# Attention stage: the second half of each token group scaled by ScalarE a head at a time, and one row moved by a transfer

## What is computed

```python
kv  = einsum('bhsd,bhse->bhde', k, v)
out = einsum('bhsd,bhde->bhse', q, kv)
rms = sqrt(mean(out * out, axis=-1, keepdims=True) + 1e-06)   # one per token and head
x   = out / rms * g_norm                                      # [8, 576, 512]
X   = fft(fft(x, axis=1), axis=2);  u = x + real(X)           # head of the second stage
# then twice: u + relu(norm(u) @ w1) @ w2, the second time after a rank-32 mix over the tokens
```

## Time and profile before

| | us |
|---|---|
| median of 3 runs (lowest, highest) | 1857.5 (1851.31, 1861.46) |
| the profiled execution, its whole time | 1865.05 |
| its span in the profile | 1862.7 |
| busy in the span: PE, DVE, ACT, POOL | 1752.5, 1387.9, 783.9, 604.2 |

### The profile page before, as it was taken

One profiled execution on the slowest core, in us unless ns is written; L12 is line 12 of the kernel. 1 busy time (PEld: TensorE's weight loads), 2 busy tenths in 40 slices (PEclk: granted clock), 3 DMA queues, 4 the chain that ended last, 5 costly groups with the idle time before them and its releaser, 6 DMA issues.

```text
span 1862.7 us, 25843 instructions
## 1 busy us (share of the span) xinstructions
PE 1752.5 (94%) x9908; PEld 1681.7 (90%) x9908; DVE 1387.9 (75%) x1559; ACT 783.9 (42%) x1126; POOL 604.2 (32%) x428
## 2 busy tenths in 40 slices
PE   5989868979999999999999999799999999999998
PEld 5767758969999999999999999789999999999998
DVE  3899975897797787877866768965956857758667
ACT  1333333634443544544444436334334434443442
POOL 2888862453041231330320213620410402303203
PEclk9999988989999999999999999899999999999999
DMA  7557548898688787787876778786676766766663
GB/s 251 182 196 237 195 155 315 307 336 295 246 299 273 258 298 270 280 290 257 295 257 232 255 244 316 285 299 221 247 241 232 240 234 245 249 226 240 228 247 122
DMA packets 123819, 470.04 MB, mean 252 GB/s; under 512 B 12273, under 2 KB 49649, under 8 KB 84018
## 3 DMA queue, kind: packets, MB, share of 16 engines
q1 hardware_dynamic: 122482, 467.21, 71.1%
q10 hardware_dynamic: 1216, 1.18, 0.2%
HBM read 389.70 MB, written 78.64 MB: 251 GB/s over the span
## 4 chain that ended last, share of the span: by engine, by line
PE 72%; DVE 15%; issue 5%; POOL 3%; DMA 3%; SPq 0%; ACT 0%; ACTq 0%; DVEq 0%; POOLq 0%
PE pair L837 11%; PE pair L839 11%; PE pair L838 11%; PE pair L854 11%; PE pair L856 11%; PE pair L855 10%; DVE t_raw L1366 3%; DVE t_lo L1347 2%; PE tr_ps L721 2%; DMA in_sb<-x_dram 1%; POOL x_sb L1527 1%; DVE eo_sb L1238 1%; DVE ce_sb L1246 1%; PE pair L628 1%; DVE ss_sb L1212 1%
## 5 line engine op out<-in xcount | busy, mean ns | idle before, releaser
L854 PE MATMUL pair<-t_hi,w_sb 128*128 128x384 f32 x1344 | 462.8, 344 | 33.8 <-DVE t_lo L1347 33.7
L837 PE MATMUL pair<-t_hi,w_sb 128*128 128x384 f32 x1344 | 462.4, 344 | 15.6 <-DVE h_sb L1384 8.3
L855 PE MATMUL pair<-t_lo,w_sb 128*128 128x384 f32 x1344 | 458.2, 341 | 0.0
L856 PE MATMUL pair<-t_hi,w_sb 128*128 128x384 f32 x1344 | 458.1, 341 | 0.0
L838 PE MATMUL pair<-t_lo,w_sb 128*128 128x384 f32 x1344 | 457.3, 340 | 0.0
L839 PE MATMUL pair<-t_hi,w_sb 128*128 128x384 f32 x1344 | 457.2, 340 | 0.0
L1347 DVE TENSOR_TENSOR t_lo<-t_raw,t_hi 128x768 fp32r<-128x768 f32 x300 | 346.4, 1162 | 11.0 <-ACT t_hi L1067 7.6
L1572 POOL TENSOR_TENSOR t_raw<-h_sb 128x768 f32<-128x768 f32 x60 | 150.4, 2507 | 573.7 <-PE pair L856 573.7
L1082 ACT ACTIVATE t_hi<-t_raw 128x768 fp32r<-128x768 f32 x240 | 202.1, 846 | 314.9 <-DVE t_raw L1366 236.4
L854 PEld LDWEIGHTS pair<-t_hi,w_sb 128*128 128x128 f32 x1344 | 254.6, 189 | 42.6 <-DVE t_lo L1347 42.3
L837 PEld LDWEIGHTS pair<-t_hi,w_sb 128*128 128x128 f32 x1344 | 254.0, 189 | 23.7 <-issue 14.1
(11 more groups left out here) (149 smaller groups left out, 2115.8 us busy)
## 6 DMA issues: line engine op xcount, KB each, us to landing
w_sb<-wc SPq DMA_DIRECT2D x260, 1024.0 KB, 4.9
wc<-w_sb SPq DMA_DIRECT2D x28, 1024.0 KB, 5.8
w_raw<-wr1a SPq DMA_DIRECT2D x24, 512.0 KB, 4.9
w_raw<-wr1b SPq DMA_DIRECT2D x24, 512.0 KB, 4.2
wc<-pb SPq DMA_DIRECT2D x16, 640.0 KB, 4.8
w_raw<-wr2a SPq DMA_DIRECT2D x10, 1024.0 KB, 7.0
wc<-pb_v SPq DMA_DIRECT2D x16, 640.0 KB, 4.8
w_raw<-wr2b SPq DMA_DIRECT2D x10, 1024.0 KB, 7.2
```

Of the source, the lines that this page charges most:

```text
L837: nc.tensor.matmul(ps, w_hi, hi[:, x, :], start=(fresh and x == 0), stop=False, skip_group_check=True)
L854: nc.tensor.matmul(ps, w_hi, hi[:, f, :], start=(fresh and k == 0 and f == 0), stop=False, skip_group_check=True)
L855: nc.tensor.matmul(ps, w_hi, lo[:, f, :], start=False, stop=False, skip_group_check=True)
L856: last = nc.tensor.matmul(ps, w_lo, hi[:, f, :], start=False, stop=(k == 3 and f == 1), skip_group_check=True)
```

## The change

Of each group's two members DVE scales only the first (m = 0). The second is scaled by ACT with eight instructions, one for each head: 96 partitions by 64 columns from PSUM to SBUF, a copy whose scale is one column of `rinv_sb`, one value for each partition. They stand in ACT's queue as `normalise(b, g)`: for g = 0 between `copy_seq` 0 and 1, for g = 1 behind root 1, for g = 2 behind root 2 and ahead of `copy_kv`. Their first instruction waits for the reciprocal (`inverted`). The semaphore `scaled` becomes two, `scaled_dve` and `scaled_act`, and all who waited for the one wait for both, but for PE's sine slot 1, which waits for DVE's alone.

The copy of the middle row (L1249) leaves DVE. ACT issues a transfer of it from `x_sb` to `mrow_sb` (`save_row`, 2 KB, SBUF to SBUF) behind `copy_g`, once `weigh` of group 0 is done; `fix_row` and the first `add_transform` of that batch wait for its landing. In batch 0, `save_row` stands ahead of `copy_kv(1)`.

```diff
             def attention(...):
                     if g == 0 and not first:
-                        pe.wait_ge(scaled, 6 * b)
+                        pe.wait_ge(scaled_dve, NT * b)
+                        pe.wait_ge(scaled_act, NT * b)
...
                     if g == 2:
-                        pe.wait_ge(scaled, 6 * b + 2)
+                        pe.wait_ge(scaled_dve, NT * b + 1)
+                        pe.wait_ge(scaled_act, NT * b + 1)
...
+            def normalise(b, g):
+
+                act.wait_ge(inverted, NT * b + g + 1)
+                if b >= 3 and g == 0:
+                    act.wait_ge(u_stored[b % 3], 16 * NT * (b // 3))
+                for h in range(H):
+                    cols = slice(HD * h, HD * (h + 1))
+                    last = nc.scalar.activation(x_sb[b % 3][:, 2 * g + 1, cols], att_ps[2 * (g % 2) + 1][0:PT, cols],
+                                                ACT.Copy, scale=rinv_sb[:, g % 2, H + h:H + h + 1])
+                last.then_inc(scaled_act, 1)
+
+            def save_row(b):
+
+                act.wait_ge(x_ready, NT * b + 1)
+                if b >= 2:
+                    act.wait_ge(row_fixed, b - 1)
+                act.dma_start(mrow_sb[:, b % 2, :], x_sb[b % 3][0:1, 1, :]).then_inc(row_saved[b % 2], 16)
...
                 root(b, 0)
-                copy_seq(b - 1, (0, 1))
+                copy_seq(b - 1, (0,))
+                normalise(b, 0)
+                copy_seq(b - 1, (1,))
                 root(b, 1)
+                normalise(b, 1)
                 copy_seq(b - 1, (2, 3))
                 copy_g(b - 1)
+                save_row(b)
                 if not first:
                     split_unit_hi(UNITS[b - 1])
                 square(b, 2, False)
                 if more:
                     root(b, 2)
+                    normalise(b, 2)
                     copy_kv(b + 1)
...
-                for m in range(2):
-                    nc.vector.tensor_tensor(
-                        x_sb[b % 3][:, 2 * g + m, :].rearrange("p (h e) -> p h e", h=H),
-                        att_ps[2 * (g % 2) + m][0:PT, :].rearrange("p (h e) -> p h e", h=H),
-                        rinv_sb[:, g % 2, H * m:H * (m + 1)].unsqueeze(2).to_broadcast([PT, H, HD]),
-                        ALU.mult).then_inc(scaled, 1)
+                nc.vector.tensor_tensor(
+                    x_sb[b % 3][:, 2 * g, :].rearrange("p (h e) -> p h e", h=H),
+                    att_ps[2 * (g % 2)][0:PT, :].rearrange("p (h e) -> p h e", h=H),
+                    rinv_sb[:, g % 2, 0:H].unsqueeze(2).to_broadcast([PT, H, HD]), ALU.mult).then_inc(scaled_dve, 1)
...
                 if g == 0:
-                    nc.vector.tensor_copy(mrow_sb[:, b % 2, :], x_sb[b % 3][0:1, 1, :])
...
             def fix_row(b):
                 dve.wait_ge(u_added, NT * b + 1)
+                dve.wait_ge(row_saved[b % 2], 16 * (b // 2 + 1))
...
             def weigh(b, g):
                 pool.wait_ge(gn_loaded, 16)
-                pool.wait_ge(scaled, 2 * (NT * b + g + 1))
+                pool.wait_ge(scaled_dve, NT * b + g + 1)
+                pool.wait_ge(scaled_act, NT * b + g + 1)
...
             def add_transform(b, t):
                 pool.wait_ge(ds_ready, NT * b + t + 1)
+                if t == 0:
+                    pool.wait_ge(row_saved[b % 2], 16 * (b // 2 + 1))
```

More of the change, by code:

```diff
@@ L306, in build_program @@
         att_done, squared, summed, eps_set = sem("att_done"), sem("squared"), sem("summed"), sem("eps_set")
-        rooted, inverted, scaled, x_ready = sem("rooted"), sem("inverted"), sem("scaled"), sem("x_ready")
+        rooted, inverted, x_ready = sem("rooted"), sem("inverted"), sem("x_ready")
+        scaled_dve, scaled_act, row_saved = sem("scaled_dve"), sem("scaled_act"), [sem(f"row_saved{n}") for n in range(2)]
         eo_ready, folded = sem("eo_ready"), sem("folded")
@@ L694, in feature_transform @@
                     if t == 1:
-                        pe.wait_ge(scaled, 6 * b + 10 if more else 6 * B)
+                        pe.wait_ge(scaled_dve, NT * (b + 1) + 2 if more else NT * B)
                     elif t or not first:
@@ L774, in up_room @@
                         pe.wait_ge(kv_copied, 2 * B)
-                        pe.wait_ge(scaled, 6 * B)
+                        pe.wait_ge(scaled_dve, NT * B)
+                        pe.wait_ge(scaled_act, NT * B)
                     elif k == 1:
@@ L1023, in _ @@
             root(0, 0)
+            normalise(0, 0)
             root(0, 1)
+            normalise(0, 1)
+            save_row(0)
             copy_kv(1)
@@ L1027, in _ @@
             root(0, 2)
+            normalise(0, 2)
             def deviation(n):
```

## The result

The kernel with the change took 1870.38 us (median of 8 runs, 1867.66 to 1875.44), the kernel before, on the same chips, 1857.59 (8 runs, 1851.31 to 1864.27). The ratio is 1.0073, with an interval of 1.0054 to 1.0093: the change makes the kernel slower by 12.8 us, where +5.7 was forecast. The time lies above the 1858 to 1869 that the forecast itself was given, in the range of 1848 to 1877 and on the slower side of the 0.5% that can be told, a side that had 0.34. The profiled execution took 1873.11, against 1865.05 before.

A forecast was written before the change was run, and what follows sets the result against it. DVE was taken as full in the attention part but held twice a step by a chain through ACT and POOL. Terms of 4.65, 0.42 and 0.60 gave +5.7 us, from 1857.5 to 1863.2, range 1848 to 1877.

The forecast's parts named there:

- PE as the bound or more stalls: Slower case: PE's slow clock delays key-value products, 1875, or DVE stalls in three steps more, 1869; chance 0.26.
- the forecast's own: The main case, a time of 1858 to 1869 us around the sum's 1863.2; chance 0.52.
- the middle row: Row copy moved from DVE to an ACT-issued transfer: -0.42 us a step, with ACT's issue of about 0.67 taken as covered.
- The price of ACT's copies: Each 96x64 copy 0.32 us long and 0.21 from start to start; eight end 1.79 after the first starts.
- Group 0: `weigh` 0 starts later behind ACT's eight copies, +0.51 us a step; DVE's saved 1.28 falls into its wait for POOL.
- Group 1: `copy_seq` 1 waits behind the eight copies, PE runs 2.3 us late, and `weigh` 1 is still on time.
- three signs of being wrong: Copies closer than 0.15 us apart, no DVE idle before L1259, or PE, not ACT, releasing the cosine copies at half clock.
- PE becomes the bound: Rival: a 1.2 GHz stretch on the key-value products delays unfold 0 about 3 us; four steps, +12, 1875; chance 0.26 with more stalls.
- Group 2: Eight copies ahead of `copy_kv` and the cosine copies: unfold 0 starts 0.84 us later, and DVE waits 1.48 there.
- The sum: Five usual steps of +0.93, step 2 +0.42, batch 0 +0.60, last step 0.0: +5.7 us, giving 1863.2.
- DVE's time comes free: Faster rival: 18.7 us leave DVE; were all of it on the path, 1838.8; chance 0.14 together with fewer stalls.
- It doesn't do what it says: Rival: the eight ACT copies cost only the lower bound, so the stage keeps its length or gains a little, 1852; chance 0.08.

The follow-up runs named there:

- g2: The changed kernel without the row's transfer, so DVE copies the row again and ACT keeps the eight copies: 1867.85 us, 1.0050 of before.
- f3: The changed kernel with ACT's `copy_seq` of token slots 1 and 2 each one place earlier, slot 1 ahead of group 0's eight copies: 1864.72 us, 1.0031 of before.
- g7: The changed kernel with DVE scaling both members again and ACT making its eight copies beside that on a scratch area, same waits: 1870.67 us, 1.0085 of before.
- g8: The changed kernel with extra PE matmuls of 200 columns ahead of token slots 1 and 2, their results overwritten: 1870.75 us, 1.0073 of before.
- h1: The kernel before with the row's transfer added into a scratch row, with all its waits, DVE's own copy kept and used: 1862.05 us, 1.0031 of before.
- h3: The changed kernel with ACT's copies of token slots 1 and 2 moved earlier and the row copied by DVE, without the transfer: 1867.28 us, 1.0054 of before.
- g0: The kernel before, unchanged, profiled once more for a second trace: 1862.49 us in that execution.
- f1: The kernel before with only the row's transfer, issued by ACT, in place of DVE's copy; scaling stays on DVE: 1862.61 us, 1.0027 of before.
- h2: The kernel before with only the row's transfer in place of DVE's copy, measured a second time: 1860.91 us, 1.0021 of before.

## Why the prediction was right or wrong, point by point

**The time.** The change came out in the range, but 7.1 us over the sum, in the part that was kept for PE as the bound or more stalls (0.26) and not in the forecast's own (0.52). By the timed halves one term of the sum makes up that distance, the middle row: -3.4 forecast, +4 to +5.5 measured. The scaling alone costs what was forecast for it, 9.3 against 9.1. That agreement is partly luck, as the terms in it were not all right: the stalls were as in before in the forecast, and g2's trace has two more of them.

**The price of ACT's copies: right.** 0.32 long and 1.79 for eight were forecast, 0.312 and 1.72 measured. The trace agrees with the forecast's own rows more than with the 0.33 and 0.24 that were estimated from the Trainium skill (ScalarE: Activation LUTs, What ACT_TABLE_LOAD costs): (1.72 - 0.312) / 7 is 0.20 from start to start. The rule of the Trainium skill (ScalarE: Activation LUTs, Rules for kernel authors) to multiply on VectorE bears out here in sign: g2, the move alone, is +0.5%.

**Group 0: right.** `weigh` 0 was forecast 4.4 to 4.5 after the first sums and starts at 4.41; this is POOL's timeline of step 3 of the kernel after.

```profile
117.39 6.40 POOL L1560 TENSOR_TENSOR x_sb<-x_sb,gn_sb 96x256 f32<-96x256 f32 x8 [1.28 <-ACT x_sb L953]
```

DVE's L1268 follows 7.21 after the first sums, before it was 6.75: +0.46, forecast +0.51. The saving of 1.28 is gone, as said: in g7 DVE gets its 15.4 us back, and the medians differ by 0.3, with the interval of 6.5 to each side.

**Group 1: wrong in steps without a stall.** "In a step without DVE's 4 us stall ACT is there 1.93 earlier, at 153.9, and PE isn't: the two come out level." A lateness of 2.3 used up all of PE's room, and nothing was left over for what came with it: PE's new pause ahead of slot 3 is followed in the trace by a stretch at 1.2 GHz (0.50 from 117.57 to 127.00, stage mean 0.88, 0.91 before), and in step 3 the matmuls got some 5 us longer by it (3.25 - 1.73, 2.95 - 1.62, 3.71 - 1.97 and 6.33 - 5.98, the last two by f3's rows). So PE was not level in unstalled steps but late: they take 29.6 to 31.8, forecast 28.7. f3 takes PE's lateness away and gets the forecast step, 28.3 to 28.6. The clock goes with the pauses in these traces, 0.92 in g8 where they are filled and 0.94 in f3 where two copies come earlier, but g8's time stayed, so what the clock alone is worth is open. Of the prediction's three signs of being wrong this is the third, and it came: in step 3 PE, with a stretch at half clock behind it, releases the copies ahead of unfold 0. The rival "PE becomes the bound" named this mechanism and its price; its chance of 0.26 was too low for a case in which the forecast's own working ended with no margin.

**Group 2: right for ACT, short for PE.** Forecast 1.48 of waiting at unfold 0; ACT's own part is 1.81 (f3, g2), the change has 1.8 to 3.6.

**The middle row: the failed term, wrong in sign.** It was set to -0.42 a batch, -3.4 in all, with the issue at nothing. In the traces a step does get 0.27 shorter. In the timed runs three kernels with the transfer cost 4.1, 5.5 and 5.3 us, by h1 because of what was added: 7.5 to 8.9 us beside the forecast, as much as the whole sum missed. Where these us go is open. The traces can't say it: the two of before are of executions 5 and 7.5 us over its median, so nearly every kernel looks as if it lost more in the timed runs than its stage explains. Counted from the span's start to the end of the stage, against the mean of the two traces of before (252.9), ten of the twelve other kernels (all but the change and g7) lose 3 to 7 us more in the timed ratio than in the trace, and g2 and h3, which have no transfer, are among them (4.8 and 5.9).

**The sum.** By batches the change's stage grew +0.6, +2.6, -0.7, +4.1, +1.4, +1.2, +2.0 and -0.8 against the first trace of before, 10.4 in all. The forecast had +0.6, then five of +0.93, +0.42 and nothing for the last. Batch 0 is right from its first sums on, but these come 1.9 us later, which was not forecast. The surplus lies where the step is without a stall: steps 1, 3, 5 and 6 grew by 9.8, against 3.7 forecast (step 6 of before was a stalled one). That is the account of one trace against one, and it doesn't add to that of the timed halves: by the trace the surplus is PE's, by the timed runs it is the row's, and f3's gain speaks for PE. How the two share it is open. The shift was carried on one for one. In the profiled runs the stage ended 12.3 later and the span only 8.6, since the rest of the span varies by some 5 us between traces whatever the kernel (1604.8 to 1610.1 in most, see the table), so single spans could not settle it.

**DVE's time comes free: fell.** It lost 26.7 us of busy time and the stage became longer. **It doesn't do what it says: fell,** the tile's view has it all.

## What to carry to other kernels

Price moved work by its length in each chain through the engine that takes it, and by everything queued behind it there, not by that engine's idle share: ACT was busy a third of the stage before (76.39 of 228), and 1.7 us in each of three places made the kernel slower. Ahead of such work put what feeds the engine that has least room, here two of the copies from PSUM that let PE go on (5.7 us). And where a working ends with "the two come out level", price the side that has no room left. A term that is small and put at nothing, like the issue of the transfer here, is the cheapest to measure alone, and it was the one that missed most.

## What the runs showed of the hardware that was not expected

- DVE's stall beside a busy POOL comes and goes in the same program: two traces of before have it in three and in two of the steps 3 to 7, at 4.09 to 4.25 us each, and in g0 a step with it is 1.95 longer.
- A transfer of 2 KB between two tiles of SBUF, issued by ACT once a batch (0.515 us of issue, landing after 2.6 us and more) and added to the kernel before costs 4 to 5.5 us over eight batches in timed runs (f1, h2, h1). With f3's order the kernel without it, h3, is no faster. The traces don't show where it goes. Each is 32 packets on its queue: 1216 became 1472.
- A short copy on ACT with a scale from a tensor, 96x64, starts 0.20 us after the one before it and lasts 0.31, and one of 96x512 lasts 0.68: eight heads as eight instructions take 2.5 times the one.
